# More matmuls without a reader in the start's waits, and another order of ScalarE's and VectorE's work at the first gate product

## The chip, the cores and the metric

The kernel runs on one core of one Trainium2 chip. The time is that of one launch in microseconds (us) on the device. TensorE (PE) does matmuls and transposes, VectorE (DVE), ScalarE (ACT) and GpSimd (POOL) work element by element, and SyncE (SP) issues the loads. The engines run side by side, each through its own instructions in a fixed order, and wait for each other on semaphores.

## The reference

Three layers follow one another. What is computed, shortened:

```python
# attention: B, H, S, D = 4, 8, 576, 64
scores = q @ k.T / sqrt(D)
mask   = local (0 <= i-j < 32) for heads 0-3, strided (i >= j, i%32 == j%32) for heads 4-7
attn   = exp(where(mask, scores, -1e9) - max); attn /= attn.sum(-1) + 1e-9
x      = (attn @ v) as [2304, 512]
# gated layer: 512 -> 1536 -> 512
xn  = x / sqrt(mean(x*x) + 1e-6) * rms_g
g   = xn @ w_gate;  val = xn @ w_val
y   = (g * sigmoid(g) * val) @ w_out
# eight experts, one per token: 512 -> 1024 -> 512
e   = argmax(y @ router_w + bias[modality]);  p = softmax(...)[e]
out = p * (relu(y @ w1[e]) @ w2[e])
```

## The kernel before, in words

Every large product is done as three matmuls on pairs of numbers (a high part in fp32r and the rest, a low part): hi·hi, hi·lo and lo·hi. So a tile that goes into such a product is first copied to its high part by ScalarE or GpSimd (`x_hi`, `gate_hi`) and then subtracted to its low part by VectorE (`x_lo`, `gate_lo`).

**Attention.** The masks leave few keys for a query, so the scores of 4 batches are cut into 56 groups of four small blocks; a batch has 14 groups. For a group `j` PE makes four score blocks (`score`, L1032, "x8" in the trace, since an fp32 matmul is shown as two), DVE adds the mask and takes the row maxima (`mask_max`, L1351), ACT takes the exponentials with their sums (`exps`, L1261), DVE inverts the sums (`invert`, L1360 and L1362), POOL multiplies (`normalise`, L906), PE transposes the weights (`turn_probs`, L1042), ACT copies them out (`evac_probs`, L1237), PE multiplies with v (`values`, L1061), and ACT copies the result O into `xT` (`evac_o`, L1253). q and k are transposed before that (`turn_qk`, L1009) and copied out by DVE (L1454) in the first stage, by ACT (L1309) later. Every group has one of four places for its tile: `sm0` to `sm2` and, for one group in four of the first stage, `sm_early`.

**The order by ticks.** Each engine's program is a loop over ticks `s`, and tables say what an engine does in a tick. The first stage is `EARLY` = 20 ticks, 0 to 19, with one group in each: these are all groups of batch 0 and the first six of batch 1. At the end of each of these ticks PE does three matmuls (four or six in ticks 16, 17 and 19) on a tile `warm` that nobody reads (`keep_busy`, L1166, bf16, 512 columns); the same is done before tick 0. From tick 20 on the gated layer runs, in 6 chunks of 384 tokens with 12 blocks of 128 hidden columns; a block has 6 ticks: gate product in two halves of six matmuls, val product in two halves, and the down product of the block before in two. The last 36 groups of attention, and the transposes of their q and k, are put between them.

**The seam between the stages.** In ticks 16 to 19 the sum of squares of the first chunk goes PE, DVE (`roots`), PE (`spread_roots`, L1084), and then DVE scales `xT` (`normalise_x`, L1405, four instructions), ACT makes `x_hi` (L1269, four) and DVE makes `x_lo` (L1412, four). The first gate product starts in tick 20. Its first half needs `x_hi` alone; the second half (tick 21) needs all four parts of `x_lo`. Ahead of this second half PE's program has two other things in tick 21: `turn_probs(17)`, which writes PSUM bank 7 and therefore waits until ACT has copied O of group 16 out of it (`s_oe`), and `turn_qk` of the first pair of batch 1, which writes bank 6, waits for DVE's `mask_max(19)` to have read the scores there (`s_m`), and waits for the load of q and k of that pair (`s_qk`). `score(20)` in tick 22 waits for ACT's copy of that transpose (`s_qe`).

Which tick a group's work has is told by `SCORE`, `EXPS`, `INVERT`, `NORM`, `TURN` and `PV`. `HEAD` is 20, so group 19 is the last one of the first stage. The other engines take from a tick's list in the order in which the functions below stand.

Of the kernel before, what the change touches and what calls it, by code (L numbers as in the profile page):

```python
# [23 lines left out]
G = B * NG  # L24
# [26 lines left out]
HEAD = 20  # L51
# [8 lines left out]
def score_tick(j):  # L60
    if j < HEAD:
        return j
    if j < 2 * NG:
        return EARLY + 2 + 3 * (j - HEAD)
    return EARLY + SPAN - 6 + 6 * (j - 2 * NG)


def by_tick(ticks):
    out = {}
    for what, s in ticks:  # L70
        out.setdefault(s, []).append(what)
    return out


SCORE = {j: score_tick(j) for j in range(G)}
# [3 lines left out]

PLACE = {j: j % SM if j < HEAD else (j - HEAD) % (SM - 1) for j in range(G)}  # L80
PRIOR = {j: max((i for i in range(j) if PLACE[i] == PLACE[j]), default=None) for j in range(G)}
EXPS = {j: SCORE[j] + (0 if j < HEAD else 1) for j in range(G)}
INVERT = {j: SCORE[j] + (1 if j < HEAD else 3) for j in range(G)}
NORM = {j: SCORE[j] + (1 if j < HEAD else 4) for j in range(G)}


def qk_ticks(b, hp):
# [11 lines left out]
PV_AT = by_tick((j, s) for j, s in PV.items())  # L99
EXPS_AT = by_tick((j, s) for j, s in EXPS.items())  # L100
INVERT_AT = by_tick((j, s) for j, s in INVERT.items())
NORM_AT = by_tick((j, s) for j, s in NORM.items())
QK_AT = by_tick((k, s) for k, s in QK.items())
# [10 lines left out]
SPREAD = {c: s + (2 if c == 0 else 6) for c, s in SS.items()}  # L114
# [38 lines left out]
def fused_kernel(nc, q, k, v, w_gate, w_val, w_out, rms_g, modality_id, router_w, router_bias, w1, w2, x2, out):  # L153
# [4 lines left out]
    with ctx:  # L158
# [211 lines left out]
        s_mr = sem("residue_mask_read")  # L370
# [592 lines left out]
        def front_pe(pe):  # L963
# [19 lines left out]
            def residues():  # L983
                pe.wait_ge(s_ms, 2)
                pe.matmul(ps[0:SQ, 4, 0:SQ], same[:, :], same[:, :], start=True, stop=True).then_inc(s_res, 1)
                pe.wait_ge(s_mr, 1)

            def turn_qk(b, hp, t):

# [173 lines left out]
            def keep_busy(n):  # L1163

                for i in range(n):
                    pe.matmul(ps[:, 3, :], warm[:, 0:P], warm[:, :], start=True, stop=True)  # L1166

            pe.wait_ge(s_warm, 1)
            keep_busy(3)
            residues()  # L1170
            pe.wait_ge(s_cst, 2)
            pe.wait_ge(s_zero, 4)
            keep_busy(6)
            for s in range(TICKS):
                if s < EARLY:
                    for key in QK_AT.get(s, []):
                        turn_qk(*key)
                for j in SCORE_AT.get(s, []):
                    score(j)
                for j in TURN_AT.get(s, []):  # L1180
                    turn_probs(j)
                for j in PV_AT.get(s, []):
                    values(j)
                if s >= EARLY:
                    for key in QK_AT.get(s, []):
                        turn_qk(*key)
                if s < EARLY:
                    keep_busy({16: 4, 17: 4, EARLY - 1: 6}.get(s, 3))
                for c in SS_AT.get(s, []):
                    sum_squares(c)  # L1190
                for c in SPREAD_AT.get(s, []):
                    spread_roots(c)
                for key in Y_AT.get(s, []):
                    turn_y(*key)
                for key in LOGITS_AT.get(s, []):
                    logits(*key)
                if s == COUNT_1:
                    early_counts(pe)
                if s == PLACE_1:
                    early_place(pe)  # L1200
                if s == ROWS_1:
                    turn_rows(pe, 0, 0)
                if s >= EARLY:
                    c, f, sub, half = step_of(s)
                    if sub == 0:
                        gate_product(c, f, half)
                    elif sub == 1:
                        val_product(c, f, half)
                    elif f:
                        down(c, f - 1, range(TT)[2 * half:2 * half + 2])  # L1210
                        if f == FT - 1 and half:
                            down(c, f)
# [115 lines left out]
        def front_dve(dve):  # L1328
# [80 lines left out]
            def x_split(c):  # L1409
                for kk in range(KT):  # L1410
                    dve.wait_ge(s_xh, KT * c + kk + 1)
                    dve.tensor_tensor(xl[:, kk, :], xT[:, kk, x_cols(c)], xh[:, kk, :].bitcast(f32),  # L1412
                                      ALU.subtract).then_inc(s_xl, 1)
# [25 lines left out]
            for s in range(TICKS):  # L1439
                c, f, sub, half = step_of(s) if s >= EARLY else (0, 0, -1, 0)  # L1440
                if (sub, half) == (1, 0):
                    scale_gate(FT * c + f)
                if (sub, half) == (2, 0):
                    form_h(FT * c + f)
                if (sub, half) == (2, 1):
                    h_split(FT * c + f)
                for x in SPREAD_AT.get(s - 1, []):
                    normalise_x(x)
                    if x == 0:
                        x_split(x)  # L1450
                if s < EARLY:
                    for key in QK_AT.get(s, []):
                        dst, src = evac_qk(dve, *key)
                        dve.tensor_copy(dst, src).then_inc(s_qe, 1)  # L1454
                for j in SCORE_AT.get(s, []):
                    mask_max(j)
                for x in SS_AT.get(s - 1, []):
                    roots(x)
                for j in INVERT_AT.get(s, []):
                    invert(j)  # L1460
                for key in LOGITS_AT.get(s, []):
                    add_bias(*key)
                for val, i in SPLIT_AT.get(s - 2, []):
                    w_lo(val, i, 1)
                for val, i in SPLIT_AT.get(s - 1, []):
                    w_lo(val, i, 0)
                if (f, sub, half) == (FT - 1, 2, 1) and c + 1 < NC:
                    x_split(c + 1)
                if s == HOT_1:
                    dve.wait_ge(s_le, EARLY_TILES)  # L1470
                    dve.wait_ge(s_tab, 10)
                    one_hot(dve, 0, EARLY_TILES)
                if s == GATE_1:
                    gates(dve, 0, 0, EARLY_TILES)
                if s == STAR_1:
                    early_expert(dve)
                if s == RANK_1:
                    early_ranks(dve)
                if s == MARK_1:
                    early_marks(dve)  # L1480
                if s == POS_1:
                    early_positions(dve)
                if s == IDX_1:
                    early_indices(dve)
                for second, i in W_SPLIT_AT.get(s - 1, []):
                    early_w_lo(dve, second, i)
                if s == ROWS_LO_1:
                    rows_lo(dve, 0)
# [437 lines left out]
```

## Time and profile before

| | |
|---|---|
| median of 3 runs | 930.12 us (929.95 to 930.21) |
| the profiled execution | 929.51 us |
| its span, first to last instruction | 927.7 us |
| mean granted TensorE clock | 0.984 |
| PE busy | 898.6 us, 97% of the span |
| DVE, ACT, POOL busy | 49%, 39%, 33% |

The span leaves out 1.8 us around the program. A busy share is an average: PE is busy in nearly all of the span, with a few short stretches where it isn't, or where its clock is down. "Granted clock" is the share of TensorE's clock pulses let through; 1.00 is 2.4 GHz and 0.50 is 1.2 GHz. The chain of waits goes back from the last instruction to what released each one. An instruction's time in the timeline includes its way through the engine, so that neighbours overlap: the step from one start to the next is the rate.

### The profile page before, as it was taken

The page shows a single profiled execution, that of the slowest core. Times are in us where ns is not written, and L with a number is a line of the kernel's source. Part 1 is how long each engine was busy: PE and PEld are TensorE (multiplying, and loading weights), DVE is VectorE, ACT ScalarE, POOL GpSimd, SP SyncE. Part 2 cuts the span into 40 slices and gives each one's busy share as a digit, 9 for nine tenths or more (in the row PEclk, how much of TensorE's full clock was granted, in tenths as well). Part 3 has the DMA queues.
Part 4 walks back from the last instruction along what each step waited for, and adds up shares of the span by engine and source line. Part 5 has one row for each costly group of instructions (what it writes and reads, how often), then busy time and mean ns, then how long its engine had stood idle before and what let it go on. Part 6 is the DMA issues. An engine that isn't in the chain of part 4 may idle for free.

```text
span 927.7 us, 15901 instructions
## 1 busy us (share of the span) xinstructions
PE 898.6 (97%) x5433; PEld 767.6 (83%) x5433; DVE 456.4 (49%) x1239; ACT 360.9 (39%) x935; POOL 308.1 (33%) x366
## 2 busy tenths in 40 slices
PE   8989999999999999999999999999789999999996
PEld 5657898888878888799999999998678888888884
DVE  5864555433454345522433343774754466446651
ACT  5866413544444444421121131242243355335430
POOL 2734762344233342344234233240502222212221
PEclk9999999999999999999999999999889999999998
DMA  8972212222113211211121121610836355515521
GB/s 180 276 188 77 58 51 65 66 65 73 49 44 107 61 27 32 67 36 36 35 80 35 39 75 35 222 51 35 302 135 242 129 182 189 201 48 197 194 74 35
DMA packets 74486, 94.95 MB, mean 102 GB/s; under 512 B 38701, under 2 KB 42797, under 8 KB 74416
## 3 DMA queue, kind: packets, MB, share of 16 engines
q1 hardware_dynamic: 70656, 82.51, 29.2%
q0 software_dynamic: 3760, 11.54, 3.6%
q8 instruction: 40, 0.66, 0.3%
q14 instruction: 30, 0.25, 0.1%
HBM read 84.59 MB, written 10.22 MB: 102 GB/s over the span
## 4 chain that ended last, share of the span: by engine, by line
PE 90%; DVE 4%; ACT 1%; issue 1%; POOL 1%; DMA 1%; ACTq 0%; POOLq 0%; DVEq 0%
PE ps L1100 34%; PE ps L1139 15%; PE ps L1575 13%; PE ps L1590 11%; PE ps L1032 3%; PE ps L1061 2%; PE ps L1602 2%; PE ps L1042 2%; PE ps L1009 2%; PE ps L1166 1%; PE ps L1159 1%; PE ps L569 1%; PE ps L1150 1%; DMA xg<-x_rows,idx_gather 1%; DVE h_lo L1429 0%
## 5 line engine op out<-in xcount | busy, mean ns | idle before, releaser
L1418 DVE SCALAR_TENSOR_TENSOR h<-h,ps 128x384 f32<-128x384 f32 x72 | 39.9, 554 | 175.2 <-ACT h L1276 175.1
L906 POOL TENSOR_TENSOR sm<-sm,rinv 72x288 f32<-72x288 f32 (+1 forms) x51 | 45.6, 894 | 204.2 <-DVE rinv L1362 204.1
L1100 PE MATMUL ps<-x_hi,gate_hi 128*128 128x384 f32 x288 | 104.1, 362 | 0.0
L1100 PE MATMUL ps<-x_hi,val_hi 128*128 128x384 f32 x288 | 102.1, 354 | 0.0
L936 POOL CAST out_hi<-out_raw 128x512 fp32r<-128x512 f32 x72 | 46.6, 648 | 155.1 <-DMA out_raw<-in_moe_w_out 155.1
L1100 PE MATMUL ps<-x_hi,gate_lo 128*128 128x384 f32 x288 | 97.5, 338 | 0.0
L938 POOL TENSOR_TENSOR out_lo<-out_raw,out_hi 128x512 fp32r<-128x512 f32 x72 | 95.1, 1322 | 5.8
L1100 PE MATMUL ps<-x_hi,val_lo 128*128 128x384 f32 x288 | 96.9, 337 | 0.0
L1100 PE MATMUL ps<-x_lo,val_hi 128*128 128x384 f32 x288 | 96.9, 336 | 0.0
L1100 PE MATMUL ps<-x_lo,gate_hi 128*128 128x384 f32 x288 | 94.4, 338 | 0.0
L1139 PE MATMUL ps<-out_hi,h_hi 128*128 128x512 f32 x216 | 89.4, 414 | 2.1 <-DVE h_lo L1429 2.1
L1429 DVE TENSOR_TENSOR h_lo<-h,h_hi 128x384 fp32r<-128x384 f32 x72 | 64.4, 895 | 43.5 <-ACT h_hi L1280 43.5
L1139 PE MATMUL ps<-out_hi,h_lo 128*128 128x512 f32 x216 | 85.3, 395 | 0.0
L1139 PE MATMUL ps<-out_lo,h_hi 128*128 128x512 f32 x216 | 84.9, 393 | 0.0
L1532 POOL DMA_INDIRECT out_rows<-yo,idx_s x21 | 21.7, 1032 | 179.0 <-DVE yo L1766 177.2
L1280 ACT ACTIVATE h_hi<-h 128x384 fp32r<-128x384 f32 x72 | 37.7, 524 | 105.6 <-DVE h L1424 105.6
L1261 ACT ACTIVATE sm<-sm,nmin 72x72 f32<-72x72 f32 (+1 forms) x204 | 73.3, 363 | 12.1 <-DVE nmin L1351 12.0
L1424 DVE SCALAR_TENSOR_TENSOR h<-h,ps 128x384 f32<-128x384 f32 x72 | 39.9, 554 | 68.5 <-PE ps L1100 68.3
L1276 ACT ACTIVATE h<-ps 128x384 f32<-128x384 f32 x72 | 34.9, 484 | 98.6 <-PE ps L1100 98.4
L1739 DVE TENSOR_TENSOR w_lo<-w_raw,w_hi 128x1024 fp32r<-128x1024 f32 x60 | 69.4, 1220 | 4.2 <-ACT w_hi L1666 4.0
L1590 PE MATMUL ps<-w_hi,hT_hi 128*128 128x512 f32 x168 | 68.1, 405 | 0.0
L1590 PE MATMUL ps<-w_lo,hT_hi 128*128 128x512 f32 x168 | 66.4, 395 | 0.0
(248 smaller groups left out, 1926.2 us busy)
## 6 DMA issues: line engine op xcount, KB each, us to landing
w_raw<-in_moe_w SPq DMA_DIRECT2D x64, 512.0 KB, 6.6
out_raw<-in_moe_w_out SPq DMA_DIRECT2D x72, 256.0 KB, 2.6
x_rows<-y_tiles SPq DMA_DIRECT2D x18, 256.0 KB, 2.4
early_w_raw<-in_moe_w SPq DMA_DIRECT2D x8, 512.0 KB, 6.1
gate_raw<-in_moe_w_gate SPq DMA_DIRECT2D x4, 768.0 KB, 9.8
val_raw<-in_moe_w_val SPq DMA_DIRECT2D x4, 768.0 KB, 9.5
qk<-in_q SPq DMA_DIRECT2D x8, 288.0 KB
qk<-in_k SPq DMA_DIRECT2D x8, 288.0 KB
```

Of the source, the lines that this page charges most:

```text
L906: pool.tensor_tensor(s3, s3, rinv[0:n, i, :].unsqueeze(2).to_broadcast([n, 4, c]), ALU.mult).then_inc(s_no, 1)
L936: pool.tensor_copy(oh[i][:, :], o_raw[i][:, :]).then_inc(s_oh, 1)
L938: pool.tensor_tensor(ol[i][:, :], o_raw[i][:, :], oh[i][:, :].bitcast(f32), ALU.subtract).then_inc(s_ol, 1)
L1100: mm = pe.matmul(ps[:, bank, 0:CH], w[:, i, kk, cols], x[:, kk, :], start=(m == 0), stop=(m == n - 1))
L1139: mm = pe.matmul(ps[:, 2 + t, :], a[:, cols], w[:, :], start=(f == 0 and i == 0), stop=(f == FT - 1 and i == 2))
L1261: act.activation(s2, s2, ACT.Exp, scale=-1.0, bias=nmin[0:n, k_, i:i + 1], accum_out=rsum[0:n, k_, i:i + 1]).then_inc(s_ex, 1)
L1418: dve.scalar_tensor_tensor(out=hf[n % 2][:, :], in0=hf[n % 2][:, :], scalar=1.0, in1=ps[:, 0, 0:CH], op0=ALU.add, op1=ALU.mult).then_inc(s ...
L1424: dve.scalar_tensor_tensor(out=hf[n % 2][:, :], in0=hf[n % 2][:, :], scalar=0.5, in1=ps[:, 1, 0:CH], op0=ALU.mult, op1=ALU.mult).then_inc( ...
L1429: dve.tensor_tensor(hl[n % 2][:, :], hf[n % 2][:, :], hh[n % 2][:, :].bitcast(f32), ALU.subtract).then_inc(s_hl, 1)
L1575: mm = pe.matmul(ps[:, half, :], x[:, kk, :], w[:, kk, half * 512:(half + 1) * 512], start=(kk == 0 and n == 0), stop=(kk == KT - 1 and n ...
L1590: mm = pe.matmul(ps[:, 5, :], x[:, j, :], w[:, j, :], start=(j == 0 and n == 0), stop=(j == FJ - 1 and n == 2))
L1739: dve.tensor_tensor(lo[:, i * n:(i + 1) * n, :], raw[:, i * n:(i + 1) * n, :], hi[:, i * n:(i + 1) * n, :].bitcast(f32), ALU.subtract).the ...
```

## The change

Three edits, all in the order of the work. No operation of the result is added or taken away.

1. At the start PE no longer waits for the mask of the residues (`s_mr`) ahead of its matmuls without a reader. There are seven of them there, not six, one more between the two pairs of q and k transposes of tick 0, and two more between those and `score(0)`.
2. Group 19's exponentials, inversion and normalisation move by a tick: `EXPS` from 19 to 20, `INVERT` and `NORM` from 20 to 21.
3. DVE's `x_split(0)` (the four `x_lo`) no longer stands right behind `normalise_x(0)`, but behind `mask_max(19)` of the same tick.

```diff
-EXPS = {j: SCORE[j] + (0 if j < HEAD else 1) for j in range(G)}
-INVERT = {j: SCORE[j] + (1 if j < HEAD else 3) for j in range(G)}
-NORM = {j: SCORE[j] + (1 if j < HEAD else 4) for j in range(G)}
+
+EXPS = {j: SCORE[j] + (0 if j < HEAD - 1 else 1) for j in range(G)}
+INVERT = {j: SCORE[j] + (1 if j < HEAD - 1 else 2 if j < HEAD else 3) for j in range(G)}
+NORM = {j: SCORE[j] + (1 if j < HEAD - 1 else 2 if j < HEAD else 4) for j in range(G)}
...
                 pe.matmul(ps[0:SQ, 4, 0:SQ], same[:, :], same[:, :], start=True, stop=True).then_inc(s_res, 1)
-                pe.wait_ge(s_mr, 1)
...
             residues()
+            keep_busy(7)
+            pe.wait_ge(s_mr, 1)
             pe.wait_ge(s_cst, 2)
             pe.wait_ge(s_zero, 4)
-            keep_busy(6)
             for s in range(TICKS):
                 if s < EARLY:
                     for key in QK_AT.get(s, []):
+                        if s == 0 and key[2] == 2:
+                            keep_busy(1)
                         turn_qk(*key)
+                if s == 0:
+                    keep_busy(2)
...
                 for x in SPREAD_AT.get(s - 1, []):
                     normalise_x(x)
-                    if x == 0:
-                        x_split(x)
...
                 for j in SCORE_AT.get(s, []):
                     mask_max(j)
+                if s == SPREAD[0] + 1:
+                    x_split(0)
```

ACT's program at the seam, before (`sm_early` is group 19's tile, `xT` under it is O of group 16, `pt` the weights of group 17):

```order
L1253 ACTIVATE xT<-ps 128x2x72 [waits pv_done]
L1269 ACTIVATE x_hi<-xT 128x384 [waits normed_x] x4
L1261 ACTIVATE sm_early,rsum<-sm_early,nmin 72x72 [waits masked_with_max] x4
L1253 ACTIVATE xT<-ps 128x2x72 [waits pv_done]
L1237 ACTIVATE pt_110<-ps 72x288 [waits pv_done,probs_transposed]
L1309 ACTIVATE qT_101<-ps 128x3x96 [waits scored,qk_transposed]
```

The same place now:

```order
L1258 ACTIVATE xT<-ps 128x2x72 [waits pv_done]
L1274 ACTIVATE x_hi<-xT 128x384 [waits normed_x] x4
L1258 ACTIVATE xT<-ps 128x2x72 [waits pv_done]
L1266 ACTIVATE sm_early,rsum<-sm_early,nmin 72x72 [waits masked_with_max] x4
L1242 ACTIVATE pt_110<-ps 72x288 [waits pv_done,probs_transposed]
L1314 ACTIVATE qT_101<-ps 128x3x96 [waits scored,qk_transposed]
```

O's copy has changed places with the four exponentials; all else stands as it stood, five lines further down in the file.

DVE's program there, before (each ISA pair is one block's mask and maximum):

```order
L1405 SCALAR_TENSOR_TENSOR xT<-xT,rms_gain,ps 128x384 x3
L1412 TENSOR_TENSOR x_lo<-xT,x_hi 128x384 [waits x_hi_split] x4
L1351 ISA sm_early,nmin<-ps,mask_str 72x72 [waits probs_transposed,scored]
L1351 ISA nmin 72x1
L1351 ISA sm_early,nmin<-ps,mask_str 72x72
```

And now:

```order
L1410 SCALAR_TENSOR_TENSOR xT<-xT,rms_gain,ps 128x384 x3
L1356 ISA sm_early,nmin<-ps,mask_str 72x72 [waits probs_transposed,scored]
L1356 ISA nmin 72x1
L1356 ISA sm_early,nmin<-ps,mask_str 72x72
L1356 ISA nmin 72x1
L1356 ISA sm_early,nmin<-ps,mask_str 72x72
L1356 ISA nmin 72x1
L1356 ISA sm_early,nmin<-ps,mask_str 72x72
L1356 ISA nmin 72x1
L1417 TENSOR_TENSOR x_lo<-xT,x_hi 128x384 [waits x_hi_split] x4
L1365 TENSOR_SCALAR rsum<-rsum 72x4 [waits exponentiated_and_summed]
L1367 RECIPROCAL rinv<-rsum 72x4 [waits eps_added]
```

The four `x_lo` have gone behind all of `mask_max(19)`, and still stand ahead of the inversion of group 18 (the last two rows).

PE's program at the start now (`warm` is the tile without a reader, `qk_93` the first pair's q and k):

```order
L1166 MATMUL ps<-warm 128x512 x2
L986 MATMUL ps<-same_residue 72x72 [waits strided_mask_made]
L1166 MATMUL ps<-warm 128x512 x7
L1009 MATMUL ps<-ident,qk_93 128x72 [waits pads_zeroed,qk_loaded2,constants_made,residue_mask_read]
L1009 MATMUL ps<-ident,qk_93 128x72 x7
L1166 MATMUL ps<-warm 128x512
L1009 MATMUL ps<-ident,qk_93 128x72 [waits qk_evacuated,qk_loaded2]
```

The wait for the residues' mask has gone from the first of these matmuls to the first transpose, and one such matmul stands between the transposes.

## Rows read from the trace of the kernel before

**Rows 1.** The page: busy time, share of the span and instructions of each engine.

```profile
PE 898.6 (97%) x5433; PEld 767.6 (83%) x5433; DVE 456.4 (49%) x1239; ACT 360.9 (39%) x935; POOL 308.1 (33%) x366
```

**Rows 2.** The chain of waits at the seam: start us, us, what.

```profile
56.10 0.97 DVE x_lo L1412 x3
...
59.62 0.32 ACT xT L1253
```

**Rows 3.** Timeline, PE: start, us, line, out<-in, idle before and releaser.

```profile
57.52 0.34 PE L1100 MATMUL ps<-x_hi,gate_hi 128*128 128x384 f32 x1
57.70 0.34 PE L1100 MATMUL ps<-x_hi,gate_lo 128*128 128x384 f32 x1
...
59.98 0.45 PE L1042 MATMUL ps<-ident,sm 72*72 72x72 f32 x4 [1.95 <-ACT xT L1253]
...
61.75 0.77 PE L1032 MATMUL ps<-kT,qT 64*72 64x72 f32 x8
```

**Rows 4.** Timeline, ACT at the seam.

```profile
55.24 1.76 ACT L1269 ACTIVATE x_hi<-xT 128x384 fp32r<-128x384 f32 x4
...
58.85 0.34 ACT L1261 ACTIVATE sm_early<-sm_early,nmin 72x72 f32<-72x72 f32 x1
...
59.19 0.34 ACT L1261 ACTIVATE sm_early<-sm_early,nmin 72x72 f32<-72x72 f32 x1
...
60.47 0.41 ACT L1237 ACTIVATE pt<-ps 72x288 f32<-72x288 f32 x1 [0.53 <-PE ps L1042]
60.77 0.72 ACT L1309 ACTIVATE qT<-ps 128x288 f32<-128x288 f32 x1
```

**Rows 5.** Timeline, DVE at the seam.

```profile
56.02 1.96 DVE L1412 TENSOR_TENSOR x_lo<-xT,x_hi 128x384 fp32r<-128x384 f32 x4
57.90 0.22 DVE L1351 CUSTOM_DVE_ANT_0 sm_early<-ps,mask_str 72x72 f32<-72x72 f32 x1
...
58.51 0.16 DVE L1360 TENSOR_SCALAR rsum<-rsum 72x4 f32<-72x4 f32 x1
```

**Rows 6.** L760's issues between 50 and 53 us: count, ns; time to landing.

```profile
L760 SPq DMA_DIRECT2D qk<-in_k x2: 1349/2307/3265, 49.5 to 50.9; - x2
...
DMA to landing us min/median/max: 6.9/7.0/7.0
```

**Rows 7.** Stretches: length, busy by engine, granted clock, DMA share, GB/s.

```profile
61.60:65.01 3.41, 3.41 (x20) 2.93 (x18) 2.05 (x10) 0.49 (x1) 2.48 (x2) 0.50 0.58 143
68.43:71.84 3.41, 1.96 (x26) 1.70 (x27) 2.26 (x12) 2.03 (x7) 0.81 (x2) 1.00 0.33 109
```

**Rows 8.** Groups of one product's matmuls, 62.4 to 64.5, then 66.4 to 67.6 us: busy, mean ns.

```profile
L1100 PE MATMUL ps<-x_hi,val_lo 128*128 128x384 f32 x2 | 1.0, 522 | 0.0
...
L1100 PE MATMUL ps<-x_hi,val_lo 128*128 128x384 f32 x2 | 0.7, 344 | 0.0
```

**Rows 9.** The chain of waits behind the seam.

```profile
65.22 0.41 ACT pt L1237
...
65.77 0.48 PE ps L1061 x8
```

**Rows 10.** Timeline, PE at the start.

```profile
2.90 0.51 PE L985 MATMUL ps<-same_residue 32*72 32x72 f32 x2
3.74 2.74 PE L1166 MATMUL ps<-warm 128*128 128x512 bf16 x6 [0.32 <-DVE mask_str L1335]
6.27 1.01 PE L1009 MATMUL ps<-ident,qk 72*128 72x72 f32 x8
7.60 0.74 PE L1009 MATMUL ps<-ident,qk 72*128 72x72 f32 x8 [0.32 <-DVE qT L1454]
8.96 0.49 PE L1032 MATMUL ps<-kT,qT 64*72 64x72 f32 x8 [0.61 <-DVE kT L1454]
9.38 0.82 PE L1166 MATMUL ps<-warm 128*128 128x512 bf16 x3
```

**Rows 11.** Stretches of 4 us further on.

```profile
668.00:672.00 4.00, 4.00 (x10) 3.13 (x11) 0.51 (x1) 0.00 (x0) 2.35 (x5) 0.50 0.95 329
```

## The prediction

> **What bounds the kernel now.** The page comes first: PE is busy in 97% of the span, no other engine in half of it [rows 1]. So a change gains only where PE stands still or runs slowly, and then nearly one to one, for PE has work queued up to the end. The chain of waits says where that is. In the first 20 ticks it stays on PE nearly throughout, leaves it once for the roots, and at the seam it runs through `x_lo`, then the exponentials, then O's copy [rows 2]. The timeline of PE shows the hole: the sixth matmul of the gate product's first half starts at 57.70, the next instruction, `turn_probs(17)`, at 59.98, with 1.95 us idle and ACT's copy of O as releaser [rows 3]. ACT is late since O's copy stands behind four exponentials, and they are late since the maxima start on DVE only at 57.90, after 1.96 us of `x_lo` [rows 4, 5].
>
> The stretches show a second loss. Right behind the hole, from 61.6 to 65.0 the granted clock is 0.50, which is 1.2 GHz, and there one of the product's matmuls takes 522 ns where it takes 344 ns a little later at 2.4 GHz [rows 7, 8]. I read the low clock as the consequence of the hole before it. The same follows once more a little later: from 68.43 to 71.84 PE is busy for 1.96 us of 3.41 [rows 7], and after that the clock is low again; the change has nothing for that one.
>
> **The seam, step by step.** I lay out what each engine does now, with the durations of before.
>
> DVE: `x_lo` started at 56.02, the place that the maxima now have; I let these start at 56.10, when the last scaling of `xT` is over by the chain [rows 2]. From first maximum to the next thing behind they took 58.51 − 57.90 = 0.61 us [rows 5]: over at 56.75. `x_lo` then needs 56.75 to 58.7.
>
> ACT: `x_hi` ends at 57.00 [rows 4]. O's copy of group 16 comes next, 0.32 us [rows 2], so bank 7 is free at about 57.35 instead of 59.94. The four exponentials follow at 0.34 us each [rows 4], until 58.75. They no longer wait for their maxima. Then the copy of group 17's weights, 0.30 from its start to the next start (60.47 to 60.77), and the copy of the transposed q, 0.72 [rows 4]: 59.75.
>
> PE: the first half's six matmuls end their issue at 57.9, and bank 7 is free. `turn_probs(17)` takes 0.25, so `turn_qk` is due at 58.15. Its maxima have been read since 56.75. Its load is the narrow place: the last of the pair's four transfers was issued at 50.9 and landed 7.0 us later, at 57.9 [rows 6]. This wait ended unseen behind the hole before; now it has 0.25 us of room. I put it at nothing. The second half of the gate product then starts at 58.4 and issues for 1.1 us; its third matmul is the first that needs `x_lo`, which by then has two parts and gets the fourth at 58.7, before the sixth matmul. So the cost of the moved `x_lo` is nothing too, with PE's own work as cover. PE is through at 59.5. `score(20)` waits for ACT's copy of q until 59.75 and starts, with the 0.14 us that such a wait takes (from 65.22 + 0.41 to 65.77 [rows 9]), at 59.9. It started at 61.75 [rows 3]. **First term: 1.85 us.**
>
> The clock. `score(20)`, the val product's first half and the transposes of group 18 stood between 61.75 and the copy at 65.22, 3.47 us at 1.2 GHz nearly throughout [rows 3, 9]. At 2.4 GHz I count 0.42 for the scores, six steps of 0.18 (from 57.52 to 57.70 [rows 3]) and 0.45 for the transposes with their way out: 1.95. **Second term: 1.5 us**, if the clock stays up. After the change the only idle time between the first half and `score(20)` is some 0.45 us ahead of the latter, where there were 1.95 in one piece. With three quarters of the hole gone I take the clock to stay up.
>
> The Trainium skill has a rule that speaks against this term: in "TensorE: Matmul & The Clock Gate", Part 4, it says that a transpose "doesn't count as PE-busy the same way". What fills the former hole begins with seven transposes, 0.5 us. By that rule the clock could fall in spite of them, and the sum would be 1.5 us smaller; no row of before separates the two.
>
> Moved behind, and what waits for it: group 18's inversion now comes after `x_lo`, at 58.7 instead of 58.51, and POOL's multiplication with it; group 18 is transposed at about 61.5. Group 19's multiplication goes behind the split of the first `out` block, about 1.9 us of POOL, to 61.9; it is wanted four ticks later. POOL's `gate_hi` behind both stays near 62.5, so DVE's `gate_lo` ends near 65.0, where `form_h(0)` would be due at 64.6. ACT's `h_hi` behind it isn't due before 65.6. No cost; here the gain of PE begins to touch DVE, and I keep 0.4 us as bound.
>
> **The start.** Three matmuls take up to 2.9, then two passes for the residues, then 0.32 us of idle, six matmuls at (6.27 − 3.74)/6 = 0.42 us, then the transposes [rows 10]. Now the seven can start right behind the residues, at about 3.2 (two short passes) or at worst 3.45, and last 2.95 us: transposes at 6.15 to 6.4 instead of 6.27. The matmul between the transposes lies in an idle time of 0.32, the two ahead of the scores in 0.61 [rows 10]. At the start's rate of 0.42 the first would not fit by 0.1 us and the two by 0.25; at the rate from 9.38 on (three in 0.82 with their way out, 0.22 each) they fit. The eight transposes from 6.27 took 1.01 and those from 7.60 only 0.74, so the clock comes up near 7 us, and the fillers stand behind that. The granted clock is printed as 1.00 there, and I trust the durations. Bounds: a gain of 0.15 to a loss of 0.55; I take zero, nearest to what the rows give with fillers at full clock. The rise itself I leave where it is: PE was already busy without a gap from 3.74 to 7.
>
> **Sum.** 1.85 + 1.5 = 3.35 us, and I take off 0.1 for the room at the load and DVE: 3.25. From the profiled execution's 929.51 (927.7 of span and 1.81 around it) that gives 926.26. The runs' median lies 0.6 above the profiled one, so it is 930.12 − 3.25 = 926.9.
>
> **What comes behind.** Everything until the end moves forward by 3.25 us, PE-bound. The second low stretch at 71.8 stays: its cause is copies on ACT between transposes and values, 0.55 us from 65.22 to 65.77 [rows 9] and like ones, which the change doesn't touch. Further low stretches stand at 638, 668 (0.50 over a whole stretch of 4 us, with 10 matmuls in it [rows 11]) and 680 us; they begin after holes or very small matmuls. Whether a hole brings the clock down seems to be close in places, so a shift of the program could add or remove one fall. From rows, one lasts 3.4 us and costs half of it where PE is busy throughout, 1.7 us [rows 7].
>
> **Rivals.**
> - *The clock falls anyway*, a little later. For it: PE still waits for ACT at 59.5 and again before `values(17)`, and what comes first into the former hole are seven short transposes. (That transposes might not hold the clock is also the rule of the Trainium skill named above.) Against it: three quarters of the idle time is gone. It would leave the first term, 930.12 − 1.85 = 928.3.
> - *One fall more goes away.* For it: the close places at 71.8 and 638. Against it: nothing touches their causes. 926.9 − 1.7 = 925.2.
> - *The seam's wait is only passed on.* The load lands later than in this profile, or `x_lo` becomes what the second half waits for. For it: 0.25 us of room. If both terms go this way, the time stays at 930. Against it: the load would have to land 1.5 us later, and it depends on queues that PE doesn't drive.
> - *Slower: clock falls at other places.* The place is the work behind 600 us, which moves by 3 us against whatever decides on the clock; at 1.7 us each, two more falls eat the gain (930.3) and three end at 932.0. It decides from the second on. For it: the close cases. Against it: what was busy stays as busy as it was.
>
> The change not doing what it says I exclude: the programs have the new order.
>
> **Chances.** Forecast 0.52, clock falls anyway 0.19, one fall fewer 0.14, passed on 0.08, slower 0.07. Without the two outermost cases the range is 924.7 to 929.2. A difference of 0.2%, 1.9 us, is about what can be told from no change. 928.3 lies right at this bound and I split it: faster by more than that 0.52 + 0.14 + 0.09 = 0.75, within 0.19, slower 0.06.
>
> **What would show it.** Right: no idle PE ahead of `turn_probs(17)`, its start near 57.9; `score(20)` near 59.9; granted clock 1.00 from 61.6 to 65; mean clock up from 0.984 by about 0.002; the first transposes within 0.2 us of 6.27; the first experts' work about 3.3 us earlier. Wrong: a DMA as releaser of `turn_qk`, `x_lo` as releaser of a gate matmul, a clock of 0.50 within ten us behind the seam at a new place, or the last stage moved by clearly more or less than the seam.

## The result and the profile after

| | runs | median us | lowest to highest |
|---|---|---|---|
| before | 20 | 927.62 | 921.42 to 944.15 |
| changed | 20 | 922.06 | 919.90 to 929.02 |

The ratio of changed to before is 0.9954, 95% interval 0.9935 to 0.9972: a gain of 4.3 us with an interval of 2.6 to 6.0. The difference of the medians is 5.6 us. (Ratios and means here and below leave out runs over 1.5% above the fastest of their kernel: twelve of the 127 of before, all over 935 us, and one of each half of the seam's edits.) Only the first three runs of before, 929.95 to 930.21, were known when the prediction was made; over twenty it has runs from 921.4 to 930.2 and one of 944.2. The profiled execution of the changed kernel took 920.47 us with a span of 918.7, against 929.51 and 927.7.

The page after, to be held against [rows 1]:

```profile
PE 892.6 (97%) x5428; PEld 763.4 (83%) x5437; DVE 458.9 (50%) x1239; ACT 360.7 (39%) x935; POOL 308.6 (34%) x366
```

PE is busy for 6.0 us less with the same work and four more matmuls (the count is lower since some records are missing from a trace): its instructions ran faster, at a mean granted clock of 0.992 in place of 0.984.

PE at the seam, timeline of the changed kernel, answering to [rows 3, 9]:

```profile
57.85 0.41 PE L1042 MATMUL ps<-ident,sm 72*72 72x72 f32 x4
58.24 0.47 PE L1009 MATMUL ps<-ident,qk 96*128 96x96 f32 x3
...
59.73 0.49 PE L1032 MATMUL ps<-kT,qT 64*72 64x72 f32 x8
...
62.30 0.47 PE L1061 MATMUL ps<-pt,vstr 72*64 72x72 f32 x8 [0.59 <-ACT pt L1242]
```

`turn_probs(17)` follows the sixth matmul without idle time, 2.13 us earlier than before; `score(20)` is 2.02 us earlier (59.73 against 61.75), and `values(17)` 3.47 us earlier (62.30 against 65.77).

ACT and DVE there, answering to [rows 4, 5]:

```profile
55.23 1.76 ACT L1274 ACTIVATE x_hi<-xT 128x384 fp32r<-128x384 f32 x4
56.89 0.47 ACT L1258 ACTIVATE xT<-ps 128x144 f32<-128x144 f32 x1
57.10 0.31 ACT L1266 ACTIVATE sm_early<-sm_early,nmin 72x72 f32<-72x72 f32 x1
...
58.74 0.73 ACT L1314 ACTIVATE qT<-ps 128x288 f32<-128x288 f32 x1
```

```profile
56.01 0.22 DVE L1356 CUSTOM_DVE_ANT_0 sm_early<-ps,mask_str 72x72 f32<-72x72 f32 x1
...
56.62 1.96 DVE L1417 TENSOR_TENSOR x_lo<-xT,x_hi 128x384 fp32r<-128x384 f32 x4
58.49 0.16 DVE L1365 TENSOR_SCALAR rsum<-rsum 72x4 f32<-72x4 f32 x1
```

O's copy stands right behind `x_hi`, and the maxima take `x_lo`'s former place, all within 0.35 us of what was laid out. The clock, in stretches of the changed kernel (length, busy by engine, granted clock, DMA share, GB/s), answering to [rows 7]:

```profile
58.00:61.40 3.40, 3.40 (x30) 2.87 (x28) 2.09 (x14) 1.97 (x7) 2.38 (x3) 1.00 1.37 199
68.08:71.49 3.41, 3.41 (x20) 2.83 (x19) 0.00 (x0) 2.46 (x12) 3.33 (x4) 0.50 0.50 138
651.76:658.59 6.83, 6.83 (x21) 5.69 (x21) 5.46 (x18) 3.17 (x3) 2.62 (x4) 0.50 1.03 393
```

The low clock behind the seam is gone, the one near 70 us stayed. Further on the two profiles differ in a way that the change doesn't explain. Before had these three low stretches there, together 17.1 us where the changed kernel has 6.8:

```profile
638.45:641.86 3.41, 3.41 (x15) 3.22 (x15) 1.45 (x8) 0.91 (x1) 0.00 (x0) 0.50 0.02 5
665.76:672.58 6.82, 5.41 (x15) 3.95 (x13) 1.50 (x3) 0.60 (x1) 4.12 (x8) 0.50 0.88 307
679.41:686.24 6.83, 6.23 (x15) 4.88 (x16) 6.31 (x7) 6.82 (x8) 0.00 (x0) 0.50 0.04 18
```

Where the 9.0 us between the two spans were gained, by the start of the same instruction in both timelines:

| place | before | changed | earlier by |
|---|---|---|---|
| `values(17)` | 65.77 | 62.30 | 3.47 |
| fifth copy of y on ACT | 629.05 | 625.46 | 3.59 |
| first down product of the experts | 646.93 | 641.71 | 5.22 |
| first product on gathered rows of slot 2 | 667.72 | 663.47 | 4.25 |
| next one | 680.01 | 673.51 | 6.50 |
| down product behind it | 689.09 | 679.79 | 9.30 |

Over 560 us nothing is added or lost. The rest, 5.4 us, comes after 629 us, at the low stretches shown.

The start, PE's timeline of the changed kernel, answering to [rows 10]:

```profile
3.35 3.17 PE L1166 MATMUL ps<-warm 128*128 128x512 bf16 x7
6.41 0.80 PE L1009 MATMUL ps<-ident,qk 72*128 72x72 f32 x8
7.04 0.38 PE L1166 MATMUL ps<-warm 128*128 128x512 bf16 x1
7.59 0.74 PE L1009 MATMUL ps<-ident,qk 72*128 72x72 f32 x8 [0.17 <-DVE qT L1457]
8.17 0.60 PE L1166 MATMUL ps<-warm 128*128 128x512 bf16 x2
8.95 0.49 PE L1032 MATMUL ps<-kT,qT 64*72 64x72 f32 x8 [0.18 <-DVE kT L1457]
```

Between these two profiles the start's edit is worth nothing, as predicted: `score(0)` at 8.95 and at 8.96. The experiments show that this holds for this pair of executions only.

### The profile page after: what moved, and what is told of

Read it like the earlier page. It is cut to its first block, busy times and chain, and to the rows that moved or that the text cites. A ratio compares the mean times of both kernels' runs of the same rounds, so it can differ in the third digit from the quotient of the medians.

```text
span 918.7 us, 15901 instructions
## 1 busy us (share of the span) xinstructions
PE 892.6 (97%) x5428; PEld 763.4 (83%) x5437; DVE 458.9 (50%) x1239; ACT 360.7 (39%) x935; POOL 308.6 (34%) x366
## 4 chain that ended last, share of the span: by engine, by line
PE 91%; DVE 4%; ACT 2%; issue 1%; POOL 1%; DVEq 0%; ACTq 0%; POOLq 0%
PE ps L1100 34%; PE ps L1139 15%; PE ps L1595 12%; PE ps L1580 12%; PE ps L1032 3%; PE ps L1061 2%; PE ps L1042 2%; PE ps L1607 2%; PE ps L1166 2%; PE ps L1009 2%; PE ps L1159 1%; PE ps L570 1%; PE ps L1150 1%; DVE w_lo L1744 1%; DVE h_lo L1434 0%
## 5 line engine op out<-in xcount | busy, mean ns | idle before, releaser
L1434 DVE TENSOR_TENSOR h_lo<-h,h_hi 128x384 fp32r<-128x384 f32 x72 | 66.3, 920 | 43.5 <-ACT h_hi L1285 43.5
L1429 DVE SCALAR_TENSOR_TENSOR h<-h,ps 128x384 f32<-128x384 f32 x72 | 39.9, 554 | 64.7 <-PE ps L1100 64.5
```

What stands on the lines that cost most here:

```text
L1429: dve.scalar_tensor_tensor(out=hf[n % 2][:, :], in0=hf[n % 2][:, :], scalar=0.5, in1=ps[:, 1, 0:CH], op0=ALU.mult, op1=ALU.mult).then_inc( ...
L1434: dve.tensor_tensor(hl[n % 2][:, :], hf[n % 2][:, :], hh[n % 2][:, :].bitcast(f32), ALU.subtract).then_inc(s_hl, 1)
```

## The experiments

The seam's edits are the second and the third of the change, the start's is the first. The theories: **A**, the whole gain is made at the seam. **C**, the start's matmuls matter in executions in which the clock comes up late. **D**, both: two sums that add up; it was formed after the first four of these runs. Every kernel was timed in five rounds beside before, on the same chip within a group.

| kernel | runs | median | mean | before's mean | ratio, 95% interval |
|---|---|---|---|---|---|
| start's edit alone | 12 | 925.71 | 926.0 | 928.6 | 0.9977 (0.9952 to 1.0002) |
| seam's edits alone | 12 | 926.05 | 926.2 | 928.6 | 0.9977 (0.9947 to 1.0007) |
| copy ahead of exponentials alone | 12 | 925.68 | 925.7 | 928.6 | 0.9962 (0.9933 to 0.9991) |
| maxima ahead of `x_lo` alone | 12 | 929.01 | 926.9 | 928.6 | 0.9981 (0.9946 to 1.0017) |
| changed, again | 12 | 921.35 | 922.1 | 928.1 | 0.9944 (0.9917 to 0.9971) |
| start's edit, hole filled | 12 | 922.85 | 923.4 | 928.1 | 0.9942 (0.9916 to 0.9968) |
| changed, waits behind filled | 8 | 921.03 | 921.1 | 928.1 | 0.9927 (0.9897 to 0.9957) |
| changed, routing's wait filled | 12 | 924.80 | 924.9 | 928.1 | 0.9960 (0.9931 to 0.9989) |
| changed, only the seven | 12 | 922.85 | 923.2 | 927.6 | 0.9942 (0.9918 to 0.9966) |
| changed, only the one and the two | 12 | 923.02 | 924.0 | 927.6 | 0.9973 (0.9942 to 1.0004) |
| the same step at the next wait | 7 | 922.05 | 921.7 | 927.6 | 0.9927 (0.9901 to 0.9953) |
| before without its six | 12 | 930.24 | 930.1 | 928.1 | 1.0017 (0.9993 to 1.0040) |

A mean over twelve runs of one kernel is uncertain by 0.6 to 1.3 us (one standard error), so the profiles have to tell the mechanisms.

### The start's edit alone

```diff
-                pe.wait_ge(s_mr, 1)
...
             residues()
+            keep_busy(7)
+            pe.wait_ge(s_mr, 1)
...
-            keep_busy(6)
...
+                        if s == 0 and key[2] == 2:
+                            keep_busy(1)
...
+                if s == 0:
+                    keep_busy(2)
```

> The start's edit alone (seven, one and two matmuls without a reader, the wait moved), the seam as before. Theory A (all of the gain is made at the seam): turn_probs(17) stays at 59.98 within 0.1 us, first transposes at 6.3 to 6.4, and the mean of the runs differs by under 0.7 us from before. Theory C (the fillers matter in executions in which the clock comes up later): in the profile nothing, but the slow tail of the runs is gone and the mean is 1 to 2 us lower. A loss of up to 0.5 us would be the fillers at half clock not fitting into the waits.

Measured: mean 2.6 us under before, highest of the twelve 929.95, where before had 17 of 35 over 930. That is more than theory C's 1 to 2 us and than A's 0.7, but the ratio's interval reaches 1.0002, so these times alone don't exclude A.

The profile has the old hole, but not at the old place:

```profile
61.30 0.44 PE L1041 MATMUL ps<-ident,sm 72*72 72x72 f32 x4 [1.93 <-ACT xT L1257]
```

`turn_probs(17)` stands at 61.30 and not at 59.98 as expected, since the clock was low from 48.70 to 52.11 us, ahead of the seam. From the first transposes of tick 4 (below) it takes 46.37 us to get there, 45.14 in before. Such a fall ahead of the seam is in six of the fourteen profiles, with the start's edit and without, and in neither of the two that the prediction and its result were read from.

### The seam's edits alone

```diff
-EXPS = {j: SCORE[j] + (0 if j < HEAD else 1) for j in range(G)}
...
+EXPS = {j: SCORE[j] + (0 if j < HEAD - 1 else 1) for j in range(G)}
...
-                    if x == 0:
-                        x_split(x)
...
+                if s == SPREAD[0] + 1:
+                    x_split(0)
```

`INVERT` and `NORM` are as in the change.

> Edits 2 and 3 alone, the start as before. Theory A: turn_probs(17) near 57.9, score(20) near 59.75, values(17) near 62.3, everything up to 620 us earlier by 3.3 to 3.6 us, and over the runs the same gain as the changed kernel within 0.7 us. Theory C: 1 to 2 us less than the changed kernel in the mean of the runs.

Measured: mean 2.5 us under before, where the two series of the changed kernel lie 4.0 and 6.0 us under the runs of before beside them. The seam alone falls short of them by about two standard errors: A is unlikely by the times, and the profile says why. Its start, with the very code of before:

```profile
3.74 2.74 PE L1166 MATMUL ps<-warm 128*128 128x512 bf16 x6 [0.32 <-DVE mask_str L1335]
6.27 1.17 PE L1009 MATMUL ps<-ident,qk 72*128 72x72 f32 x8
7.60 1.19 PE L1009 MATMUL ps<-ident,qk 72*128 72x72 f32 x8 [0.16 <-DVE qT L1452]
9.34 0.77 PE L1032 MATMUL ps<-kT,qT 64*72 64x72 f32 x8 [0.55 <-DVE kT L1452]
...
10.04 1.46 PE L1166 MATMUL ps<-warm 128*128 128x512 bf16 x3
...
18.02 0.41 PE L1009 MATMUL ps<-ident,qk_of_pair 96*128 96x96 f32 x3
```

The second eight transposes take 1.19 us, not 0.74 as in [rows 10], and three matmuls at 10.04 still 1.46 instead of 0.82. TensorE works at 1.2 GHz for longer, and the first transposes of tick 4 (`qk_of_pair`) stand at 18.02 us. In the profile of before they stood at 14.84. So the code of before has executions that lose 3.2 us here, and the one profile that the prediction had was not of them. That is not all that this execution lost: the clock fell ahead of the seam too,

```profile
53.22:60.05 6.83, 6.50 (x36) 3.32 (x35) 3.82 (x25) 3.72 (x19) 1.32 (x2) 0.50 1.05 282
```

and from tick 4's transposes to `turn_probs(17)` it takes 45.88 us, 2.85 more than the 43.03 of the changed kernel. Four other profiles with one low stretch of 3.4 us there, that of the start's edit among them, lose 1.2 to 1.3 us by the same measure; the sixth (maxima first) has nothing to be held against. The seam itself went as laid out: `turn_probs(17)` at 63.90 and `score(20)` at 65.63, 1.73 us apart as before, without a hole ahead (1.88 in the changed kernel).

### Each half of the seam alone

Copy first is the first of these edits (with `INVERT` and `NORM` as in the change), maxima first the second, each on the kernel before:

```diff
-EXPS = {j: SCORE[j] + (0 if j < HEAD else 1) for j in range(G)}
...
+EXPS = {j: SCORE[j] + (0 if j < HEAD - 1 else 1) for j in range(G)}
```

```diff
-                    if x == 0:
-                        x_split(x)
...
+                if s == SPREAD[0] + 1:
+                    x_split(0)
```

> Edit 2 alone: O's copy ahead of the exponentials, x_lo still ahead of the maxima. By the step sum: turn_probs(17) at 57.9, turn_qk waits for the maxima until 58.65, gate product through at 60.0, exponentials only from 58.16, so ACT's copy of q ends at 60.4 and score(20) starts at 60.6: 1.15 us gained ahead of it. Idle PE is cut in two pieces of about 0.5 us, so the clock stays up and 1.5 us come on top: 2.6 us. If the clock falls, 1.1 us.

> Edit 3 alone: maxima ahead of x_lo, O's copy still behind the exponentials. By the step sum: exponentials from 57.0, O's copy over at 58.75, turn_probs(17) at 58.8, score(20) at about 60.45: 1.3 us gained ahead of it. 0.9 us of idle PE in one piece instead of 2.0: if the clock stays up 1.5 us on top (2.8 us), if it falls 1.3 us. Together with the run of edit 2 alone: either edit alone gives most of the gain through the clock, and the two sums don't add up to the whole.

The waits came where the sums had put them. Copy first:

```profile
59.75 0.41 PE L1042 MATMUL ps<-ident,sm 72*72 72x72 f32 x4
60.62 0.44 PE L1009 MATMUL ps<-ident,qk 96*128 96x96 f32 x3 [0.46 <-DVE nmin L1351]
62.52 0.49 PE L1032 MATMUL ps<-kT,qT 64*72 64x72 f32 x8 [0.39 <-ACT qT L1309]
```

Maxima first:

```profile
63.49 0.44 PE L1042 MATMUL ps<-ident,sm 72*72 72x72 f32 x4 [0.70 <-ACT xT L1253]
```

One leaves the wait for the maxima (0.46 us) and for ACT's copy of q (0.39), the other 0.70 us of the old wait for O's copy. In both profiles the clock behind the seam stayed up. Either half takes most of the hole, and the timed ratios can't tell them apart.

### The hole filled in place of removed

To the start's edit, with the seam's order as before, this is added:

```diff
                 for j in SCORE_AT.get(s, []):
                     score(j)
+                if s == EARLY + 1:
+                    keep_busy(8)
                 for j in TURN_AT.get(s, []):
```

> The start's edit, the seam's order as before, and eight matmuls without a reader (1.74 us) put into the seam's hole ahead of turn_probs(17): the wait stays, the idle time goes. If the low clock behind the seam comes from the hole, the seam costs its wait alone: mean about 1.5 us under e1_start times the share of executions in which the clock fell there, and score(20) to values(17) 2.5 us apart in place of 4.0. If the fall has another cause, no difference from e1_start, or 0.1 us slower.

```profile
57.93 1.90 PE L1165 MATMUL ps<-warm 128*128 128x512 bf16 x8
60.05 0.44 PE L1041 MATMUL ps<-ident,sm 72*72 72x72 f32 x4 [0.22 <-ACT xT L1259]
...
61.75 0.49 PE L1031 MATMUL ps<-kT,qT 64*72 64x72 f32 x8
...
64.32 0.47 PE L1060 MATMUL ps<-pt,vstr 72*64 72x72 f32 x8 [0.59 <-ACT pt L1243]
```

`score(20)` at 61.75 as before, `values(17)` 2.57 us behind it instead of 4.02. Nothing was reordered at the seam; only PE wasn't idle. This isolates the second term: 1.45 us, predicted 1.5, and its cause, in one profile against the three that have the hole. The mean is 2.6 us under that of the start's edit alone, taken on another chip, so with more than 0.9 us of uncertainty.

### The changed kernel again, and fillers behind the seam

> The changed kernel once more, beside before on the same chip. Theory D (two sums: the start's edit saves about 3 us in the mean since before often gets its clock late, the seam 3.3 us): mean 6 to 8 us under before, and the runs lie within 10 us of each other where those of before spread over 20. Theory A (seam alone): 3.5 us under before.

Mean 922.1 against 928.1: 6.0 us (5.2 by the ratio, 2.7 to 7.7), and the start's and the seam's edits alone gave 2.6 and 2.5 (2.1 each by the ratios). The runs spread over 7.7 us, those of before beside them over 19.3. That is what theory D says; A's 3.5 us still lies in the interval, so the sum of the two is supported by the times, not proved by them. (In the profile the transposes of tick 4 stand at 14.41.)

Matmuls in the waits behind the seam, added to the changed kernel:

```diff
+                if s == EARLY + 5:
+                    keep_busy(5)
                 for j in SCORE_AT.get(s, []):
                     score(j)
...
+                if s in (EARLY + 3, EARLY + 5):
+                    keep_busy(2)
                 for j in PV_AT.get(s, []):
```

> The changed kernel with matmuls without a reader in PE's next three waits behind the seam (two ahead of values(17), five ahead of score(21), two ahead of values(18)). If idle PE is what brings the clock down at about 70 us, it doesn't fall there any more: 1.7 us less in the executions in which it did, the mean 1 to 1.7 us under the changed kernel. If transposes and copies around it are the cause, no gain and 0.1 to 0.3 us of cost.

```profile
66.00:70.00 4.00, 3.85 (x38) 2.97 (x38) 1.16 (x11) 2.92 (x13) 2.64 (x4) 1.00 0.23 59
70.00:74.00 4.00, 3.98 (x31) 3.45 (x30) 2.49 (x12) 2.13 (x6) 2.11 (x2) 1.00 0.39 96
```

The low clock near 70 us is gone in this profile (0.76 and 0.81 in the same stretches of the changed one). It is gone in that of the next-wait kernel below too, which also has matmuls in these waits, and there in all twelve profiles without them, where it begins between 67.2 and 76.3 us. So the waits there do bring the clock down. What that is worth in time is less clear: the mean is 1.0 us under the changed kernel's of the same group, with an uncertainty of 0.8: likely, not shown. This kernel is with the next-wait kernel the fastest of the series, 0.7% under before.

### The routing's wait filled

```diff
             turn_h(1)
+            for i in range(7):
+                pe.matmul(ps[:, 0, :], e2h[:, 0, 0:P], e2h[:, 0, :], start=True, stop=True)
             pe.wait_ge(s_car, 6)
```

> The changed kernel with seven matmuls of 128x512 without a reader in PE's wait for the routing's payload (about 1.7 us idle at 648 to 650 us in the changed kernel). If this hole starts the low clock of 652 to 658.6 us, which then lasts over a stretch in which PE is busy, the mean falls by 1 to 3 us. If the small matmuls and the later holes (waits for gathered rows) are enough by themselves, under 0.5 us either way.

```profile
652.00:656.00 4.00, 3.94 (x25) 3.48 (x26) 3.66 (x10) 2.77 (x3) 0.25 (x1) 1.00 0.95 343
663.67:667.08 3.41, 2.94 (x7) 2.36 (x8) 1.23 (x3) 0.00 (x0) 2.48 (x4) 0.50 1.00 338
```

The clock stays up from 652 to 656 here, and falls at the next wait instead, the one for the gathered rows. So the wait for the payload did start the low clock of 652 us, yet there is no gain, against the 1 to 3 us expected for that case; the mean is 2.8 us above the changed kernel's of its group. A part of that was visible in its profile and is not the filler's: another low stretch, at 49 us, one of the six ahead of the seam. Where the rest comes from stays open.

### Which of the start's matmuls

Both are the changed kernel less a part. Only the seven (less the one and the two):

```diff
-                        if s == 0 and key[2] == 2:
-                            keep_busy(1)
...
-                if s == 0:
-                    keep_busy(2)
```

Only the one and the two (the seven and their place given back for the six):

```diff
-            keep_busy(7)
             pe.wait_ge(s_mr, 1)
...
+            keep_busy(6)
```

> The changed kernel without the one and the two matmuls between the transposes and the scores; the seven that start right behind the residues stay. If closing the gap of 0.3 us ahead of them is what makes the clock come up early, the mean stays at 922 to 923 us and no run is over 930. If the fillers in the later waits are needed, late starts come back: mean 924 to 927, single runs over 930 us.

> The changed kernel with the six matmuls and their wait as before, and the one and the two matmuls in the waits of tick 0 kept. If these three are what matters, mean 922 to 923 us and no run over 930. If the gap ahead of the six matters, mean 924 to 927 and single runs over 930. Each of the two possibly does half.

Neither gives a clear answer in time: 923.2 and 924.0 against 922.1 and 922.9 of the two series of the changed kernel. The profile of the seven alone shows what the fillers are for:

```profile
7.08 0.74 PE L1009 MATMUL ps<-ident,qk 72*128 72x72 f32 x8 [0.39 <-DVE qT L1453]
8.44 0.49 PE L1032 MATMUL ps<-kT,qT 64*72 64x72 f32 x8 [0.62 <-DVE kT L1453]
8.86 1.46 PE L1166 MATMUL ps<-warm 128*128 128x512 bf16 x3
```

The clock had come up before 7 us, and by the granted clock it fell back at 8.8 behind the two waits of 0.39 and 0.62 us. The transposes of tick 4 stand at 15.84. Waits of this size don't always do it: in the profile of before they are 0.32 and 0.61 us [rows 10], and the clock stayed up. The other half, the six as before with the one and the two, had its clock up early in its one profile:

```profile
15.16 0.41 PE L1009 MATMUL ps<-ident,qk_of_pair 96*128 96x96 f32 x3
```

So one profile each is against the seven alone and for the fillers alone; and the one run over 930 us (930.78) is of the fillers alone. How the 2.2 us are shared between the two stays open.

### The same step at the next wait

```diff
-EXPS = {j: SCORE[j] + (0 if j < HEAD - 1 else 1) for j in range(G)}
+EXPS = {j: SCORE[j] + (0 if j < HEAD - 1 else 3 if j == HEAD else 1) for j in range(G)}
```

`INVERT` and `NORM` of group 20 go a tick later as well, and two, one and two matmuls without a reader stand in the waits behind the seam. The kernel is otherwise the changed one.

> The changed kernel with the same step once more: group 20's exponentials go behind ACT's copy of the transposed k, for which score(21) waits 1.33 us; a few matmuls without a reader (two, one, two) in the waits that are left. By the step sum score(21) starts at 64.6 in place of 65.84, so 1.2 us less; with the low clock at about 68 us gone in most executions up to 1.7 us more. Mean 919.5 to 921.5 us. If group 20's weights come too late then (they are transposed four ticks later), the gain is given back there.

```profile
58.78 0.47 PE L1009 MATMUL ps<-ident,qk 96*128 96x96 f32 x3 [0.42 <-DMA qk<-in_k]
...
60.28 0.49 PE L1032 MATMUL ps<-kT,qT 64*72 64x72 f32 x8
...
64.64 0.41 PE L1009 MATMUL ps<-ident,qk 96*128 96x96 f32 x3
...
65.93 0.49 PE L1032 MATMUL ps<-kT,qT 64*72 64x72 f32 x8 [0.66 <-ACT kT L1318]
```

From `score(20)` to `score(21)` it takes 5.65 us, 6.11 in the changed kernel: 0.46 gained, not 1.2, and the mean of 921.7 lies just above the 919.5 to 921.5 expected. I had overlooked that ACT's copy can't start before PE's own transposes of k, at 64.64; the exponentials hid only the last part of that wait. The first row shows something else that matters: here `turn_qk` did wait 0.42 us for the load.

### Before without its six matmuls

```diff
             pe.wait_ge(s_zero, 4)
-            keep_busy(6)
```

> The kernel before without its six matmuls ahead of the first transposes; nothing else changed. The first transposes can start as soon as q and k have landed (5.9 us at the latest) in place of 6.27, which by itself would be 0.4 us faster. Theory D (before loses its time at the start to a clock that comes up late or falls back, and the slow tail of its runs is the same thing at its worst): the clock comes up at 12 us or later in the profile, matmuls of 512 columns at 0.42 us from start to start in several ticks, mean 3 us or more above before, and more runs over 935 us than one in ten. If the tail comes from elsewhere (transfers, the later stages): mean within 1 us of before and the same share over 935.

```profile
6.25 1.19 PE L1009 MATMUL ps<-ident,qk 72*128 72x72 f32 x8 [2.84 <-DMA qk<-in_k]
...
15.67 1.46 PE L1166 MATMUL ps<-warm 128*128 128x512 bf16 x3
...
19.18 0.41 PE L1009 MATMUL ps<-ident,qk_of_pair 96*128 96x96 f32 x3
```

Idle for 2.84 us, then at 1.2 GHz until past 17 us, and 4.3 us late at tick 4. The clock came up as late as D has it, but the mean is 2.0 us above before where 3 or more were expected, with the ratio's interval from 0.9993 to 1.0040, and no run is over 935, where D expected more than one in ten. The 17 runs of before beside it have none over 935 either, so this group says little on the very slow runs: a late clock at the start doesn't make them by itself, and their cause stays open. Over all groups twelve of 127 runs of before are over 935 us, and none of the 83 with the whole start's edit (highest 929.95). So that edit seems to remove them; why isn't shown.

## Why the prediction was wrong, and where it was right

The forecast was 926.9 us with a range of 924.7 to 929.2, and the median is 922.06. Step by step:

- **The first term was right.** Predicted 1.85 us at `score(20)`, measured 2.02. That `x_lo` behind the maxima costs nothing and that DVE just keeps up was seen. Two details came out otherwise. `score(20)` didn't wait for ACT's copy of q, which was over at 59.47; PE itself was through only at 59.73 and went on without idle time. And the load's 0.25 us of room was not there: the last of its transfers was issued at 51.8 and landed 6.3 to 6.4 us later, near 58.15, and `turn_qk` started 0.39 us behind `turn_probs(17)`, where five other profiles (the repeat among them) have 0.25 or 0.26. The cost was 0.14 us, about the 0.1 that the sum took off, and in the next-wait kernel's execution 0.42.
- **The second term was right**, 1.5 predicted and 3.47 − 2.02 = 1.45 measured, with the cause shown by the filled hole. The rival that the clock falls anyway fell too, as far as profiles go: in all three with the hole as it was the clock falls within 3 us of its end (at 61.6, 62.35 and 66.0 us: before, the start's edit alone, and the kernel without the six, whose seam is later), and in none of the eleven others within 3 us of the same place. The Trainium skill says in "TensorE: Matmul & The Clock Gate", Part 4, that a transpose "doesn't count as PE-busy the same way". The fall that the prediction took as possible by this rule didn't come: with seven transposes at the head of the former hole the granted clock was 1.00 from 58.00 to 61.40 us. Whether transposes hold the clock less well than matmuls no run here isolates.
- **The step on the start failed**: "Bounds: a gain of 0.15 to a loss of 0.55; I take zero". It took the clock's rise near 7 us for a property of the kernel. With the start's code of before the transposes of tick 4 stand at 14.84, 18.02, 16.75 and 18.32 us in four profiles, on average 16.98; with the whole edit at 14.82, 14.93, 14.41, 14.92, 14.63, 15.14 and 14.92, on average 14.82. So the term is some 2.2 us in the mean and not 0, an estimate from four profiles against seven, and the first four range over 3.5 us. The times agree: 2.6 us for the edit alone, with an uncertainty of 0.8. The Trainium skill says of the clock's warm-up in "TensorE: Matmul & The Clock Gate", Part 1, that "it's run-variable". The trace agrees, with the 14.84 to 18.32 us of the same code. That was to be had beforehand, and would have widened the range.
- **"Everything until the end moves forward"** was right up to 629 us. Behind that, the low stretches moved: five falls before 900 us in the profile of before, two in that of the changed kernel, and in the profiles of the other kernels between two and six. The forecast had this as rivals of one fall more or less, at 1.7 us each. The difference accounts for 5.4 of the 9.0 us between the two profiles; that so many fewer falls came with this execution is its own luck and says nothing on the change.
- **The level** was off by 2.5 us: three runs at 930.1 were taken for the kernel's time, whose median over twenty is 927.62.

Of the 4.8 us between the forecast and the measured median, 2.5 are the level and, as an estimate, 2.2 the start and 0.2 the seam. The falls ahead of the seam, at 1.2 to 2.85 us each in six other executions' profiles, are a further term, for which the prediction had no row.

As a ratio the forecast, 926.9/930.12 = 0.9965, lies within the measured interval of 0.9935 to 0.9972, but the repeat of the changed kernel (0.9944) points to its far side. With 3.5 for the seam and 2.2 for the start the sum is 5.7 us. The ratios give 4.3 (2.6 to 6.0) for the first series and 5.2 (2.7 to 7.7) for the repeat, so the sum is at the upper side of what was measured, and 3.5 for the seam alone isn't excluded by the times.

## What to carry to other kernels

When engines' orders make a hole on the bounding engine, lay out all engines' instructions behind it with their measured durations: here the starts came out within about 0.35 us. The hole of 1.95 us on PE cost twice, once by itself and once by the clock behind it, and matmuls without a reader took the second part away where the wait was left in. But one profile shows one course of the clock: read from several executions what the clock did before putting zero for an edit that keeps PE busy, and take no run-to-run spread of three runs for the kernel's own.

## What the runs showed of the hardware

- With the code of before at the start, TensorE left 1.2 GHz at about 7 us in one execution and between 12 and 16 us in three others. The printed granted clock was 1.00 all the while; only the durations tell (128x512 bf16 from start to start: 0.42 and then 0.22 us).
- A clock already up fell back after waits of 0.39 and 0.62 us with small matmuls around them, in one execution, and not after 0.32 and 0.61 us in the same places in another (before); with the waits filled, in none of seven profiles.
- The clock fell within 3 us behind a hole of 1.93 to 1.97 us on PE in three of three profiles, and not with 1.74 us of it filled, in one. It fell between 67.2 and 76.3 us in twelve of twelve profiles with waits of up to 1.3 us there, and in neither of the two with matmuls in them.
- A low stretch ahead of the seam, with the waits there the same, is in six of fourteen profiles (beginning between 48.7 and 53.5 us).
- Of the falls behind 630 us, where waits and small matmuls stand between the products, one profile shows between one and four, with the same code there in all but one kernel. Low clock up to 900 us adds up to 23.9 us in the profile of before and to 10.2 in that of the changed kernel.
